# One float32 transformer block on one core: the first MLP product as seven quarter products, on blocks of 768 tokens

## Chip, core and metric

One NeuronCore of a Trainium2 chip runs the whole program. The metric is the device time of one execution in microseconds (us); lower is better. TensorE is called PE below, VectorE DVE, ScalarE ACT, GpSimd POOL; SP (SyncE) only issues transfers.

## What is computed

The reference, cut to its core:

```python
attn = windowed_attention(q, k, v)              # B, H, S, D = 4, 8, 576, 64; window 128, a slope per head
x = attn.transpose(0, 2, 1, 3).reshape(2304, 512)
h = np.maximum(x @ w_in1, 0); x = (h * h) @ w_out1        # w_in 512 x 2048, w_out 2048 x 512
h = x @ w_in2; out = (h * np.cos(h)) @ w_out2
```

All of it is float32. The two MLPs are called layer 1 (relu squared) and layer 2 (h cos h).

## The kernel before

Attention runs first, a pair of heads at a time, 16 pairs, each in a step of a software pipeline. It leaves x transposed on chip: 128 features by 2304 tokens in each of four slabs.

Both MLPs work on blocks of N = 384 tokens, six a layer. Precision is kept by splitting every operand in two fp32r parts: hi (rounded) and lo (the rest). Each product is then three matmuls, hi*hi, hi*lo and lo*hi, summed in PSUM. All of w_in and w_out lies on chip as hi and lo (win_hi, win_lo, wout_hi, wout_lo). The weights of layer 1 are split by POOL during and just after attention, those of layer 2 in place while the last block of layer 1 uses them up (split_weight, L321 to L325: one TENSOR_SCALAR for hi, one TENSOR_TENSOR for lo). Between these two stretches POOL has nothing to do.

A block takes FT = 16 steps f, one for each 128 columns of w_in:

- PE: hidden(t, f), L486 to L499: 4 slabs x 3 = 12 matmuls of 384 columns into one of four PSUM banks. Three steps later second_product (L501 to L533): in layer 1, 12 matmuls of 384 columns; in layer 2, 9 matmuls of 512 columns (tokens are then the output's partitions). They sum over all f in four Y banks.
- Layer 1, relu_step: ACT takes relu of the PSUM tile (L607), DVE multiplies (L780), ACT rounds to g_hi (L602), DVE subtracts to g_lo (L773).
- Layer 2, cos_step: DVE reduces the angle in four instructions (L804, L806, L811, L814; L806 works on what L804 left, L814 on what L811 left), ACT takes Abs and Sin (L624, L626), DVE multiplies by h (L790), ACT rounds (L602), DVE subtracts (L773). L804, L790 and L811 read h from PSUM. The DVE work of two neighbouring f is interleaved in the order written.
- split_x (L591, L764) splits the next block's x; put_y and put_out copy Y to x, whose place SP stores to HBM in layer 2.

Each engine runs its list in the order written; semaphores join them. The order on DVE and ACT was written by hand.

Of the kernel before, what the change touches and what calls it, by code (L numbers as in the profile page):

```python
# [70 lines left out]
ACT_PIECES = [p for p in PIECES if p[0] != 1]  # L71
DVE_PIECES = [p for p in PIECES if p[0] == 1]
# [11 lines left out]
def attention_mlp_kernel(nc, q_t, k_t, v, w_in1, w_out1, w_in2, w_out2, out):  # L84
    with ExitStack() as ctx:
# [21 lines left out]
        wout_raw = place("wout_raw", [P, FT, DM], F32, wout_at)
        wout_end = top[0]

        xs = place("xs", [P, 2, 2, DT, N], F32R)  # L110
        rest_at = [top[0] - 2 * 4 * DT * N]
        rest_end = top[0]
        g_hi = place("g_hi", [P, HID_RING, N], F32R)
        g_lo = place("g_lo", [P, HID_RING, N], F32R)
        work1 = place("work1", [P, 2, N], F32)
        work2 = place("work2", [P, 2, N], F32)
# [5 lines left out]
        probs0 = place("probs0", [P, UNITS, BAND], F32, hi_at)
        pt0 = place("pt0", [P, PT_COLS], F32, hi_at)
        v_raw = place("v_raw", [P, V_RING, 2, 2, 4, D], F32, hi_at)
        v_first = place("v_first", [P, V_RING, D], F32, hi_at)
        slopes = place("slopes", [P, 8], F32, hi_at)
        distance = place("distance", [P, BAND + P], F32, hi_at)
        assert hi_at[0] <= lo_at[0]
        q_raw = place("q_raw", [P, QK_RING, S], F32, lo_at)
        k_raw = place("k_raw", [P, QK_RING, S], F32, lo_at)  # L130
# [17 lines left out]
        H_BANK, Y_BANK = 0, 4  # L148
# [768 lines left out]
```

## Time and profile before

| | us |
|---|---|
| median of three runs | 912.71 (912.64 to 913.2) |
| the profiled execution, its own time | 912.75 |
| its span, first to last instruction | 910.6 |
| PE busy in the span | 894.9 |
| DVE busy | 518.6 |
| ACT busy | 369.2 |
| POOL busy | 193.7 |

Attention fills about the first 110 us, layer 1 goes on to about 510 us, layer 2 to the end. Busy time of an engine says how full it is, not whether anything waits for it; the groups further down are read for that. Durations of single instructions are start to end. Where an engine takes independent instructions one after the other, the next one starts before the record of the last one ends.

### The profile page before, as it was taken

What the parts mean: (1) busy time and instruction counts of PE and PEld (TensorE: products, weight loads), DVE (VectorE), ACT (ScalarE), POOL (GpSimd) and SP (SyncE); (2) the same over time, 40 slices, a digit from 0 to 9 for tenths busy, and PEclk for the clock granted to TensorE, in tenths of its full rate; (3) what the DMA queues carried; (4) which work ended last, traced back from release to release, by engine and by line L of the source; (5) the groups of instructions that cost most, each with busy time, mean ns of one, the idle gap of its engine ahead of it and who ended that gap; (6) DMA issues with size and microseconds to landing.
All of it is one profiled execution on the core that took longest, in us unless ns stands there. A gap on an engine that the chain in (4) does not pass through costs nothing.

```text
span 910.6 us, 17307 instructions
## 1 busy us (share of the span) xinstructions
PE 894.9 (98%) x6128; PEld 840.7 (92%) x6128; DVE 518.6 (57%) x1239; ACT 369.2 (41%) x886; POOL 193.7 (21%) x298
## 2 busy tenths in 40 slices
PE   6999899999999999999999999999999999999998
PEld 4888799999999999999999989999999899999987
DVE  6888553333333332332353878777676776777675
ACT  7888232223232222222232344444444443443433
POOL 9888992000000000000069910000000000000000
PEclk9999999999999999999999999999999999999999
DMA  7776520000000000000134200100100100100101
GB/s 245 251 248 199 165 70 1 1 0 0 0 0 0 0 0 0 0 0 0 46 117 128 80 2 1 35 0 0 35 0 0 35 0 0 35 0 0 35 1 35
DMA packets 22922, 40.15 MB, mean 44 GB/s; under 512 B 3680, under 2 KB 8800, under 8 KB 22880
## 3 DMA queue, kind: packets, MB, share of 16 engines
q1 hardware_dynamic: 22016, 38.77, 13.1%
q10 hardware_dynamic: 864, 0.82, 0.3%
q8 instruction: 26, 0.43, 0.2%
q14 instruction: 16, 0.13, 0.0%
HBM read 34.87 MB, written 4.72 MB: 43 GB/s over the span
## 4 chain that ended last, share of the span: by engine, by line
PE 95%; DVE 2%; POOL 2%; issue 1%; ACT 0%; DVEq 0%; ACTq 0%; POOLq 0%
PE psum L497 43%; PE psum L531 22%; PE psum L516 21%; PE psum L458 4%; PE psum L416 3%; PE psum L370 2%; POOL probs L319 1%; PE psum L379 0%; DVE g_lo L773 0%; DVE work L811 0%; DVE pt L750 0%; POOL win_lo L325 0%; DVE work L804 0%; DVE work L814 0%; POOL bias L309 0%
## 5 line engine op out<-in xcount | busy, mean ns | idle before, releaser
L497 PE MATMUL psum<-xs,win_hi 128*128 (+1 forms) x1536 | 391.6, 335 | 0.0
L497 PEld LDWEIGHTS psum<-xs,win_hi 128*128 128x128 f32 x1536 | 279.4, 188 | 8.4
L497 PE MATMUL psum<-xs,win_lo 128*128 (+1 forms) x768 | 257.8, 336 | 0.0
L602 ACT ACTIVATE g_hi<-work 128x384 fp32r<-128x384 f32 x192 | 101.0, 526 | 218.6 <-DVE work L790 153.9
L773 DVE TENSOR_TENSOR g_lo<-work,g_hi 128x384 fp32r<-128x384 f32 x192 | 119.2, 621 | 57.4 <-ACT g_hi L602 57.4
L780 DVE SCALAR_TENSOR_TENSOR work<-psum,work 128x384 f32<-128x384 f32 x96 | 53.4, 557 | 170.6 <-ACT work L607 170.3
L497 PEld LDWEIGHTS psum<-xs,win_lo 128*128 128x128 f32 x768 | 144.1, 188 | 0.0
L531 PE MATMUL psum<-g_hi,wout_hi 128*128 128x384 f32 x384 | 128.3, 334 | 0.0
L531 PE MATMUL psum<-g_lo,wout_hi 128*128 128x384 f32 x384 | 128.3, 334 | 0.0
L531 PE MATMUL psum<-g_hi,wout_lo 128*128 128x384 f32 x384 | 128.3, 334 | 0.0
L607 ACT ACTIVATE work<-psum 128x384 f32<-128x384 f32 x96 | 47.1, 491 | 193.2 <-PE psum L497 193.2
L516 PE MATMUL psum<-wout_hi,g_lo 128*128 128x512 f32 x288 | 113.9, 396 | 0.0
L516 PE MATMUL psum<-wout_lo,g_hi 128*128 128x512 f32 x288 | 113.7, 395 | 0.0
L516 PE MATMUL psum<-wout_hi,g_hi 128*128 128x512 f32 x288 | 112.0, 389 | 0.3 <-DVE g_lo L773 0.3
L323 POOL TENSOR_SCALAR win_hi<-win_raw 128x512 fp32r<-128x512 f32 x32 | 21.1, 659 | 317.7 <-DMA win_raw<-w_in 317.7
L804 DVE TENSOR_SCALAR work<-psum 128x384 f32<-128x384 f32 x96 | 53.2, 554 | 52.5 <-PE psum L497 52.0
L624 ACT ACTIVATE work<-work 128x384 f32<-128x384 f32 x96 | 50.5, 526 | 57.7 <-DVE work L814 57.7
L531 PEld LDWEIGHTS psum<-g_hi,wout_hi 128*128 128x128 f32 x384 | 72.1, 188 | 0.0
L531 PEld LDWEIGHTS psum<-g_lo,wout_hi 128*128 128x128 f32 x384 | 72.1, 188 | 0.0
L531 PEld LDWEIGHTS psum<-g_hi,wout_lo 128*128 128x128 f32 x384 | 72.1, 188 | 0.0
L579 ACT ACTIVATE probs<-probs,neg_max 128x192 f32<-128x192 f32 (+1 forms) x144 | 61.8, 432 | 12.7 <-DVE neg_max L730 12.7
L516 PEld LDWEIGHTS psum<-wout_hi,g_lo 128*128 128x128 f32 x288 | 54.0, 187 | 11.5
(60 smaller groups left out, 955.5 us busy)
## 6 DMA issues: line engine op xcount, KB each, us to landing
win_raw<-w_in SPq DMA_DIRECT2D x32, 256.0 KB, 3.3
v_raw<-v SPq DMA_DIRECT2D x16, 512.0 KB, 3.2
wout_raw<-w_out SPq DMA_DIRECT2D x32, 256.0 KB, 3.3
q_raw<-q_t SPq DMA_DIRECT2D x15, 288.0 KB, 3.5
k_raw<-k_t SPq DMA_DIRECT2D x15, 288.0 KB, 4.7
out<-x SPq DMA_DIRECT2D x10, 192.0 KB, 1.9
out<-x SPq DMA_DIRECT2D x12, 128.0 KB, 1.7
out<-x SPq DMA_DIRECT2D x10, 64.0 KB, 1.6
```

Source lines behind the costliest of these rows:

```text
L416: return pe.transpose(o[:, at:at + P], of, ident[:])
L458: return pe.matmul(psum[D * h:D * h + D, O_BANK + n % 2, HALF * (n // 2):HALF * (n // 2) + HALF], block, m[block.base_partition():block.ba ...
L497: last = pe.matmul(o, wi[:, f, w], xs[:, bass.ds(par, 1), part, k, :], start=(k == 0 and n == 0), stop=(k == DT - 1 and n == 2))
L516: last = pe.matmul(psum[:, Y_BANK + c, :], g[:, r, tok], w[:, f, :], start=(first and n == 0), stop=(final and n == 2))
L531: last = pe.matmul(psum[:, Y_BANK + d, 0:N], wo[:, f, w], g[:, r, :], start=(first and n == 0), stop=(final and n == 2))
L579: act.activation(m, m, ACT.Exp, bias=neg_max[:, r, u:u + 1], scale=-1.0, accum_out=row_sum[:, r, u:u + 1]).then_inc(exp_ready, 1)
L602: act.activation(g_hi[:, f % HID_RING, :], work2[:, f % 2, :], ACT.Copy).then_inc(g_hi_ready, 1)
L607: act.activation(work1[:, f % 2, :], psum[:, H_BANK + f % HID_RING, 0:N], ACT.Relu)\
L624: act.activation(a, a, ACT.Abs).then_inc(abs_ready, 1)
L773: dve.tensor_tensor(g_lo[:, f % HID_RING, :], work2[:, f % 2, :], g_hi[:, f % HID_RING, :].bitcast(F32), ALU.subtract).then_inc(g_ready, 1)
L780: dve.scalar_tensor_tensor(out=work2[:, f % 2, :], in0=psum[:, H_BANK + f % HID_RING, 0:N], scalar=0.0, in1=work1[:, f % 2, :], op0=ALU.ma ...
L804: dve.tensor_scalar(k, h, 1.0 / (2.0 * math.pi), ROUNDER, ALU.mult, ALU.add).then_inc(angle_steps, 1)
```

## The change

**The product.** x times w_in is now made by Strassen's scheme in Winograd's form. A step n takes a super block of N = 768 tokens (SUPERS = 3 a layer) and two slabs of 128 hidden columns, j and j + 8 (STEPS = 8). w_in's part of the step is cut in quarters A11, A12, A21, A22 (256 input features by 128 hidden columns), x in quarters B11, B12, B21, B22 (256 features by 384 tokens). Seven products (PRODUCTS) of two 128-row slabs each, three matmuls a slab, 384 columns: 42 matmuls of 384 columns a step, 48 steps in all. The four quarter results come from sums of these: some are summed in PSUM, in two banks (H_BANK, i % 2), the rest by five DVE additions of PSUM and an SBUF tile (sum_of) and two ACT copies (copy_part, copy_first_sum). h now lies in SBUF (hidden_sum).

**Operands.** The sums of quarters of x (T1 to T4) are made by DVE (moving_sum, 768 columns each), rounded by ACT (round_moving), their lo parts by DVE (split_moving), once a super block and spread over the steps of the one before. The sums of w_in's quarters (S1 to S4) are made by POOL in each step, rounded by ACT, and their lo parts made by POOL.

**Weights.** Nothing of the weights stays on chip. Each step loads w_in's four quarters (load_raw) and two slabs of w_out (load_wout) again from HBM, and POOL and ACT split them again: for a step POOL has four TENSOR_TENSORs of 256 columns (weight_sums), one of 768 (weights_lo), one of 1024 (sums_lo) and two of 512 (split_wout); ACT has Copies of 768, 1024 and twice 512 columns.

**Order.** PE cuts the second products in pieces (c) and puts them between the seven products by a table (pieces_after). In layer 1 a piece is three matmuls of 512 columns and three of 256, eight a step; in layer 2 it is three of 512, twelve a step. ACT and DVE follow lists of their own (mlp_step). The first MLP step's operands are prepared within attention. At the end three second products (q = 93, 95, 94) are left.

Core of the diff, added lines only (the old functions of these names go):

```diff
+SUPERS = TOKENS // N
+STEPS = FT // 2
+ALL = 2 * SUPERS * STEPS
+W_RING = 4
+FINAL = 2 * ALL - 2
+H_BANK, Y_BANK = 0, 2
+PRODUCTS = ["A11*B11", "S2*T2", "A12*B21", "S3*T3", "S1*T1", "A22*T4", "S4*B22"]
+COMB = ["A22", "A11", "A12", "S1", "S2", "S3", "S4"]
+MOVING = [name.split("*")[1] for name in PRODUCTS]
+MOVING_LO = {"T2": 0, "T3": 1, "T4": 2}
+PLACE = {"B11": (0, 0), "T1": (0, 1), "B12": (0, 1), "B21": (2, 0), "B22": (2, 1)}
+T_STEPS = {"T3": 1, "B11": 2, "T1": 2, "T2": 3, "T4": 4, "B21": 4, "B22": 4}
...
+            def load_raw(n):
+                r, j = n % 2, n % STEPS
+                w_in = w_in2 if second(n) else w_in1
+                if n >= 2:
+                    sp.wait_ge(comb_ready, 2 * (n - 1))
+                sp.dma_start(raw[:, r, 0:2, :], w_in[j + STEPS]).then_inc(raw_landed[r], 16)
+                sp.dma_start(raw[:, r, 2:4, :], w_in[j]).then_inc(raw_landed[r], 16)
+            def load_wout(q):
+                w_out = w_out2 if second(q // 2) else w_out1
+                if q >= W_RING:
+                    sp.wait_ge(second_done, q - W_RING + 1)
+                sp.dma_start(wout_raw[:, q % W_RING, :], w_out[slab(q)]).then_inc(wout_landed[q % W_RING], 16)
...
+            def weight_sums(n):
+                r = n % 2
+                a21, a22, a11, a12 = (raw[:, r, i, :] for i in range(4))
+                pool.wait_ge(raw_landed[r], 32 * (n // 2 + 1))
+                if n > 0:
+                    pool.wait_ge(comb_ready, 2 * n)
+                pool.tensor_tensor(sums[:, 0, :], a21, a22, ALU.add).then_inc(sums_ready, 1)
+                pool.tensor_tensor(sums[:, 2, :], a11, a21, ALU.subtract).then_inc(sums_ready, 1)
+                pool.wait_ge(sums_ready, 4 * n + 1)
+                pool.tensor_tensor(sums[:, 1, :], sums[:, 0, :], a11, ALU.subtract).then_inc(sums_ready, 1)
+                pool.wait_ge(sums_ready, 4 * n + 3)
+                pool.tensor_tensor(sums[:, 3, :], a12, sums[:, 1, :], ALU.subtract).then_inc(sums_ready, 1)
...
+            def weights_lo(n):
+                r = n % 2
+                pool.wait_ge(comb_hi_ready, 2 * n + 1)
+                pool.tensor_tensor(comb_lo[:, r, 0:3, :], raw[:, r, 1:4, :], comb_hi[:, r, 0:3, :].bitcast(F32),
+                                   ALU.subtract).then_inc(comb_ready, 1)
+            def sums_lo(n):
+                r = n % 2
+                pool.wait_ge(comb_hi_ready, 2 * n + 2)
+                pool.tensor_tensor(comb_lo[:, r, 3:7, :], sums[:], comb_hi[:, r, 3:7, :].bitcast(F32),
+                                   ALU.subtract).then_inc(comb_ready, 1)
+            def split_wout(q):
+                r = q % W_RING
+                pool.wait_ge(wout_hi_ready, q + 1)
+                pool.tensor_tensor(wout_lo[:, r, :], wout_raw[:, r, :], wout_hi[:, r, :].bitcast(F32), ALU.subtract)\
+                    .then_inc(wout_ready, 1)
...
+                more = n + 1 < ALL
+                if more:
+                    weight_sums(n + 1)
+                    weights_lo(n + 1)
+                if n > 0:
+                    split_wout(2 * n - 1)
+                if more:
+                    sums_lo(n + 1)
+                split_wout(2 * n)
+            split_wout(2 * ALL - 1)
...
+            def hidden_product(n, i):
+                t, r = n // STEPS, n % 2
+                weight, moving = PRODUCTS[i].split("*")
+                w, m = COMB.index(weight), moving
+                if i < 2:
+                    pe.wait_ge(comb_ready, 2 * n + i + 1)
+                if n % STEPS == 0:
+                    pe.wait_ge(xt_ready, len(MOVING) * t + i + 1)
+                if i == 0 and n > 0:
+                    pe.wait_ge(sum_done, 5 * n)
+                elif i == 2:
+                    pe.wait_ge(part_a_ready, n + 1)
+                elif i == 3:
+                    pe.wait_ge(sum_done, 5 * n + 1)
+                elif i == 4:
+                    pe.wait_ge(first_sum_ready, n + 1)
+                elif i == 5:
+                    pe.wait_ge(sum_done, 5 * n + 2)
+                elif i == 6:
+                    pe.wait_ge(sum_done, 5 * n + 3)
+                first = i in (0, 1, 4)
+                for k in range(2):
+                    cols = slice(k * P, k * P + P)
...
+            def second_product(q):
+                n, r = q // 2, q % W_RING
+                t, start = n // STEPS, q % (2 * STEPS) == 0
+                final = q == FINAL
+                wo, wl = wout_hi[:, r, :], wout_lo[:, r, :]
+                for c in range(6 if second(n) else 4):
+                    if c == 0:
+                        pe.wait_ge(wout_ready, q + 1)
+                        pe.wait_ge(g_ready, 4 * n + (3 if q % 2 else 4))
...
...
+            def pieces_after(n, i):
+                later = second((2 * n - 3) // 2) if i < 4 else second(n - 1)
+                if n % STEPS == 1:
+                    return ((3, 3, 0, 0, 0, 0, 6) if later else (2, 2, 0, 0, 0, 0, 4))[i]
+                return ((2, 1, 2, 1, 2, 2, 2) if later else (1, 1, 1, 1, 1, 1, 2))[i]
+            def mlp_step(n):
+                earlier = second_product(2 * n - 3) if n >= 2 else iter(())
+                later = second_product(2 * n - 2) if n >= 1 else iter(())
+                for i in range(len(PRODUCTS)):
+                    hidden_product(n, i)
+                    for _ in range(pieces_after(n, i)):
+                        next(earlier if i < 4 else later, None)
...
+            def copy_part(n):
+                act.wait_ge(product_done, 7 * n + 1)
+                act.activation(part_a[:], psum[:, H_BANK, 0:NH], ACT.Copy).then_inc(part_a_ready, 1)
+            def copy_first_sum(n):
+                act.wait_ge(product_done, 7 * n + 3)
+                if n > 0:
+                    act.wait_ge(g_done, 4 * (n - 1) + 1)
+                act.activation(hidden_sum[:, 0, :], psum[:, H_BANK, 0:NH], ACT.Copy).then_inc(first_sum_ready, 1)
...
+            def weights_hi(n):
+                r = n % 2
+                act.wait_ge(raw_landed[r], 32 * (n // 2 + 1))
+                if n >= 2:
+                    act.wait_ge(product_done, 7 * (n - 1))
+                act.activation(comb_hi[:, r, 0:3, :], raw[:, r, 1:4, :], ACT.Copy).then_inc(comb_hi_ready, 1)
+            def sums_hi(n):
+                act.wait_ge(sums_ready, 4 * (n + 1))
+                act.activation(comb_hi[:, n % 2, 3:7, :], sums[:], ACT.Copy).then_inc(comb_hi_ready, 1)
...
+            def mlp_step(n):
+                t, j = divmod(n, STEPS)
+                if n > 0:
+                    cosine(n - 1, 3)
+                    if n < ALL:
+                        copy_part(n)
+                    round_g(n - 1, 2)
+                    round_wout(2 * n - 1)
+                if n + 1 < ALL:
+                    weights_hi(n + 1)
+                if n > 0:
+                    round_g(n - 1, 3)
+                if j == 1 and t > 0:
+                    (put_out(t - 1, False) if t > SUPERS else put_y(t - 1))
+                if n == ALL:
+                    return
+                copy_first_sum(n)
+                cosine(n, 0)
+                if n + 1 < ALL:
+                    sums_hi(n + 1)
+                round_g(n, 0)
+                round_wout(2 * n)
+                cosine(n, 1)
+                if t + 1 < 2 * SUPERS:
+                    for name in HI_AT[j]:
+                        round_moving(t + 1, name)
+                round_g(n, 1)
+                cosine(n, 2)
...
+                dve.tensor_tensor(moving_raw(t, name), moving_raw(t, left), moving_raw(t, right), ALU.subtract)\
+                    .then_inc(t_done, 1)
...
+            def sum_of(n, product, bank, left, to):
+                dve.wait_ge(product_done, 7 * n + product + 1)
+                dve.tensor_tensor(to, psum[:, H_BANK + bank, 0:NH], left, ALU.add).then_inc(sum_done, 1)
...
+            def angle(n, i):
+                if not second(n):
+                    return
+                h, k, w = hidden_sum[:, i, :], work1[:, i % 2, :], work2[:, i % 2, :]
+                done = 3 * (4 * (n - ALL // 2) + i)
+                if i == 0:
+                    dve.wait_ge(first_sum_ready, n + 1)
+                else:
+                    dve.wait_ge(sum_done, 5 * n + SUMS_AFTER[i])
+                dve.wait_ge(g_done, 4 * n + i - 1)
                 dve.tensor_scalar(k, h, 1.0 / (2.0 * math.pi), ROUNDER, ALU.mult, ALU.add).then_inc(angle_steps, 1)
+                dve.wait_ge(angle_steps, done + 1)
                 dve.tensor_scalar(k, k, -ROUNDER, None, ALU.add).then_inc(angle_steps, 1)
+                dve.wait_ge(angle_steps, done + 2)
...
+                dve.wait_ge(angle_steps, done + 3)
                 dve.scalar_tensor_tensor(out=k, in0=k, scalar=-TURN_LO, in1=w, op0=ALU.mult, op1=ALU.add)\
                     .then_inc(angle_ready, 1)
...
+            def make_g(n, i):
+                h, w = hidden_sum[:, i, :], work2[:, i % 2, :]
+                if second(n):
+                    dve.wait_ge(cos_ready, 4 * (n - ALL // 2) + i + 1)
+                    dve.tensor_tensor(w, h, work1[:, i % 2, :], ALU.mult).then_inc(g_done, 1)
...
+            def mlp_step(n):
+                t, j = divmod(n, STEPS)
+                if 0 < n < ALL:
+                    part_b_sum(n)
+                if n > 0:
+                    make_g(n - 1, 3)
+                    lo_g(n - 1, 2)
+                if j == 1 and t > 0:
+                    (put_out(t - 1, False) if t > SUPERS else put_y(t - 1))
+                if n < ALL:
+                    angle(n, 0)
+                    part_c_sum(n)
+                if n > 0:
+                    lo_g(n - 1, 3)
+                if n == ALL:
+                    return
+                if t + 1 < 2 * SUPERS:
+                    for name in T_AT[j] if j < len(T_AT) else ():
+                        moving_sum(t + 1, name)
+                    for name in LO_AT[j]:
+                        split_moving(t + 1, name)
+                make_g(n, 0)
+                c22_sum(n)
+                angle(n, 1)
+                lo_g(n, 0)
+                c21_sum(n)
+                make_g(n, 1)
+                angle(n, 2)
+                c12_sum(n)
+                lo_g(n, 1)
+                make_g(n, 2)
+                angle(n, 3)
...
```

## Rows read from the trace of the kernel before

**Rows 1.** The page's first part: busy time of each engine.
```profile
PE 894.9 (98%) x6128; PEld 840.7 (92%) x6128; DVE 518.6 (57%) x1239; ACT 369.2 (41%) x886; POOL 193.7 (21%) x298
```

**Rows 2.** The page's fourth part: the chain that ended last, by engine.
```profile
PE 95%; DVE 2%; POOL 2%; issue 1%; ACT 0%; DVEq 0%; ACTq 0%; POOLq 0%
```

**Rows 3.** Windows (stretch, length, then busy us and count by engine, clock, DMA).
```profile
200.00:300.00 100.00, 100.00 (x579) 100.00 (x578) 31.06 (x56) 27.56 (x56) 0.00 (x0) 1.00 0.00 0
600.00:700.00 100.00, 100.00 (x503) 90.57 (x502) 72.28 (x154) 43.79 (x83) 0.00 (x0) 1.00 0.02 8
```

**Rows 4.** The chain in order of time (start, us, what): runs of matmuls.
```profile
540.47 2.10 PE psum L497 x12
...
898.44 8.22 PE psum L516 x36
```

**Rows 5.** TensorE's timeline in attention, matmuls and their weight loads.
```profile
62.88 0.77 PE L416 MATMUL psum<-ident,probs 128*128 128x128 f32 x5
...
62.87 0.53 PEld L416 LDWEIGHTS psum<-ident,probs 128*128 128x128 f32 x5
```

**Rows 6.** VectorE's timeline (start, us) in layer 2 with POOL idle.
```profile
701.79 0.56 DVE L804 TENSOR_SCALAR work<-psum 128x384 f32<-128x384 f32 x1 [1.25 <-PE psum L497]
702.38 0.36 DVE L806 TENSOR_SCALAR work<-work 128x384 f32<-128x384 f32 x1
702.66 0.55 DVE L790 TENSOR_TENSOR work<-psum,work 128x384 f32<-128x384 f32 x1
703.13 0.54 DVE L811 SCALAR_TENSOR_TENSOR work<-work,psum 128x384 f32<-128x384 f32 x1
703.71 0.56 DVE L814 SCALAR_TENSOR_TENSOR work<-work,work 128x384 f32<-128x384 f32 x1
704.18 0.55 DVE L773 TENSOR_TENSOR g_lo<-work,g_hi 128x384 fp32r<-128x384 f32 x1
```

**Rows 7.** ScalarE's timeline in layer 2: Abs, Sin, and a Copy behind them.
```profile
528.47 0.53 ACT L624 ACTIVATE work<-work 128x384 f32<-128x384 f32 x1 [1.19 <-DVE work L814]
529.03 0.62 ACT L626 ACTIVATE work<-work,half_pi 128x384 f32<-128x384 f32 x1
529.55 0.51 ACT L591 ACTIVATE xs<-x  x1
```

**Rows 8.** Groups by form (count, busy us, mean ns, idle before): ACT copies from PSUM.
```profile
L607 ACT ACTIVATE work<-psum 128x384 f32<-128x384 f32 x96 | 47.1, 491 | 193.2 <-PE psum L497 193.2
...
L588 ACT ACTIVATE pt<-psum 128x512 f32<-128x512 f32 x16 | 9.2, 578 | 9.2 <-PE psum L416 9.2
```

**Rows 9.** VectorE's timeline in layer 2 while POOL splits weights.
```profile
518.09 1.30 DVE L814 SCALAR_TENSOR_TENSOR work<-work,work 128x384 f32<-128x384 f32 x1
519.32 0.96 DVE L773 TENSOR_TENSOR g_lo<-work,g_hi 128x384 fp32r<-128x384 f32 x1
520.20 0.55 DVE L804 TENSOR_SCALAR work<-psum 128x384 f32<-128x384 f32 x1
520.78 0.87 DVE L806 TENSOR_SCALAR work<-work 128x384 f32<-128x384 f32 x1
```

**Rows 10.** POOL's timeline in the same stretch.
```profile
517.69 1.29 POOL L325 TENSOR_TENSOR wout_lo<-wout_raw,wout_hi 128x512 fp32r<-128x512 f32 x1
518.95 0.93 POOL L323 TENSOR_SCALAR wout_hi<-wout_raw 128x512 fp32r<-128x512 f32 x1
519.96 1.48 POOL L325 TENSOR_TENSOR wout_lo<-wout_raw,wout_hi 128x512 fp32r<-128x512 f32 x1
521.40 0.73 POOL L323 TENSOR_SCALAR wout_hi<-wout_raw 128x512 fp32r<-128x512 f32 x1
```

**Rows 11.** Windows: one DVE round of that stretch.
```profile
518.09:522.61 4.52, 4.52 (x25) 4.04 (x24) 4.45 (x6) 1.67 (x4) 4.35 (x5) 1.00 0.00 0
```

**Rows 12.** Windows early in attention (columns as in rows 3).
```profile
16.00:18.00 2.00, 1.19 (x13) 0.94 (x17) 0.68 (x2) 2.00 (x10) 2.00 (x6) 0.84 1.04 391
18.00:20.00 2.00, 2.00 (x34) 1.60 (x28) 0.69 (x5) 1.70 (x7) 1.92 (x5) 0.50 0.42 154
```

More of the change, by code:

```diff
@@ L107, in attention_mlp_kernel @@
[L107 to L116, printed above, removed]
+        x_lo = place("x_lo", [P, DT, TOKENS], F32R, x_at)
+        raw = place("raw", [P, 2, 4, 256], F32)
@@ L122, in attention_mlp_kernel @@
[L122 to L130, printed above, removed]
@@ L484, in values @@
                 last.then_inc(pv_done, 1)
-            def hidden(t, f, second):
-                pe.wait_ge(win_ready, FT * second + f + 1)
-                pe.wait_ge(g_done, step(t, f, 1))
-                o = psum[:, H_BANK + f % HID_RING, 0:N]
-                par = t % 2
-                for k in range(DT):
-                    if f == 0:
-                        pe.wait_ge(xs_ready, t * DT + (k + 1))
-                    w = slice(k * P, k * P + P)
-                    for n, (wi, part) in enumerate(((win_hi, 0), (win_hi, 1), (win_lo, 0))):
-                        last = pe.matmul(o, wi[:, f, w], xs[:, bass.ds(par, 1), part, k, :],
-                                         start=(k == 0 and n == 0), stop=(k == DT - 1 and n == 2))
-                last.then_inc(h_ready, 1)
@@ L640, in put_out @@
+            def put_out(t, final):
+                at = t % SUPERS * N
                 if not final:
-                    act.wait_ge(y_done, step(t, FT - 1, 1 + HID_RING))
-                for c, col, slab, off, w in ACT_PIECES:
+                    act.wait_ge(second_done, 2 * STEPS * (t + 1))
+                for c, col, strip, off, w in ACT_PIECES:
                     if final:
-                        act.wait_ge(last_ready, c + 1)
-                    act.activation(x[:, slab, bass.ds((t - BLOCKS) * N + off, w)], psum[:, Y_BANK + c, col:col + w],
-                                   ACT.Copy).then_inc(out_act, 1)
+                        act.wait_ge(y_done, c + 1)
+                    act.activation(x[:, strip, at + off:at + off + w], psum[:, Y_BANK + c, col:col + w],
+                                   ACT.Copy).then_inc(y_act, 1)
@@ new lines, in part_b_sum, with part_c_sum, c22_sum, c21_sum @@
+            def part_b_sum(n):
+                dve.wait_ge(part_a_ready, n + 1)
+                sum_of(n, 1, 1, part_a[:], part_b[:])
+            def part_c_sum(n):
+                sum_of(n, 3, 1, part_a[:], part_c[:])
+            def c22_sum(n):
+                dve.wait_ge(sum_done, 5 * n + 2)
+                sum_of(n, 4, 0, part_c[:], hidden_sum[:, 1, :])
+            def c21_sum(n):
+                sum_of(n, 5, 1, part_a[:], hidden_sum[:, 2, :])
+            def c12_sum(n):
+                sum_of(n, 6, 0, part_b[:], hidden_sum[:, 3, :])
@@ new lines, in put_out @@
+            def put_out(t, final):
+                at = t % SUPERS * N
+                if not final:
+                    dve.wait_ge(second_done, 2 * STEPS * (t + 1))
+                for c, col, strip, off, w in DVE_PIECES:
+                    if final and c < 5:
+                        dve.wait_ge(y_done, c + 1)
+                    elif final:
+                        dve.wait_ge(second_done, 2 * ALL)
+                    dve.tensor_copy(x[:, strip, at + off:at + off + w], psum[:, Y_BANK + c, col:col + w]).then_inc(y_dve, 1)
```

566 lines of the change are left out of this document (260 added, 306 removed).

## The prediction, made before the changed kernel was run

> **What bounds the kernel now.** First the page's busy shares: PE is busy 98% of the span, DVE 57%, ACT 41%, POOL 21% [rows 1]. Then the chain of waits, which says whether that is a bound: 95% of the chain is PE [rows 2]. Then the windows by stage: in layer 1 and in layer 2 PE is busy 100 of 100 us at full clock, with 579 and 503 matmuls [rows 3]. So a matmul taken off PE is worth its full time, as long as nothing else becomes late. What can become late is read from the same rows: in layer 2 DVE already has 72 of 100 us, and that with POOL doing nothing. 100/579 is 0.173 us for a matmul of 384 columns (12 in 2.10 us on the chain [rows 4]). Layer 2 runs 12 of these and 9 of 512 columns in turn: 21 x 100/503 = 4.17, less 12 x 0.173, leaves 0.233 each; at the end 36 take 8.22, 0.228 each [rows 4]. I take 0.232.
>
> **What goes.** Before, the first products are 192 x 12 = 2304 matmuls of 384 columns, after it 48 x 42 = 2016. 288 x 0.173 = 49.8 us. The second products keep their columns. From the profiled execution's 912.75 us (the median is 912.71) that makes 863 us, if PE never waits.
>
> **256 columns.** In layer 1, 576 matmuls of 512 and 576 of 256 columns replace 1152 of 384. By columns a 256 takes 0.116 and nothing changes. The other end is 0.173, the closest spacing at which fp32r weight loads are seen (578 in 100 us [rows 3]): 576 x 0.057 = 33 us. The five transposes of 128 columns, each with a full weight load, take 0.77 us, their loads 0.53 [rows 5]; less 0.28 and 0.14 for the last one's own length, estimates, that is some 0.12 and 0.10 apart. This row is nearest to a 256, so I take 0 and keep 33.
>
> **A step of PE.** 42 x 0.173 = 7.3, and second products 24 x 0.232 + 24 x 0.116, or 36 x 0.232, = 8.35: 15.6 us in either layer, where the same work took 16.7 before (4 x 4.17). A product is 1.04, a piece 1.04 in layer 1 and 0.70 in layer 2.
>
> **DVE in layer 2, POOL set aside.** Prices from the quiet timeline [rows 6]: an independent instruction of 384 columns starts 0.47 after the one before it (L790 to L811); one that needs the result before it 0.58; SBUF to SBUF with one input (L806) lasts 0.36. So an angle, now all in SBUF and each instruction needing the last, is 0.39 + 0.39 + 0.58 + 0.57 = 1.93. An operation of 768 columns is 0.47 + 0.40 = 0.87; there are 11 in eight steps, 1.2 a step. On ACT, Abs and Sin end 1.2 after the angle and the Copy behind them starts 0.1 before that [rows 7]; Copies are 0.49 for 384 and 0.58 for 512 columns [rows 8], so an estimated 0.8 for 768 and 1.0 for 1024.
> Now the two lists, from the end of angle(n-1, 3) as 0. DVE has nothing until part_b_sum(n), which needs copy_part, which ACT's list puts behind cosine(n-1, 3): it ends at 1.6. part_b_sum, make_g and lo_g run to 3.1. angle(n, 0) needs copy_first_sum, behind round_g, round_wout, weights_hi and round_g on ACT: 4.15. The angle ends at 6.1; part_c_sum, lo_g, moving work, make_g and c22_sum at 9.2; angle 1 at 11.1; lo_g and c21_sum, then make_g(n, 1) waits for the cosine until 12.35; angle 2 ends at 14.75; c12_sum, lo_g; make_g(n, 2) waits until 16.0; angle 3 ends at **18.4**. This chain of DVE and ACT alone is longer than PE's 15.6 and than the 16.7 of before. PE is ahead of it everywhere.
>
> **POOL, which now works all the time.** Rows 9 and 10 show what that does. While POOL's TENSOR_TENSOR runs from 517.69 to 518.98, L814 takes 1.30 instead of 0.56 and ends 0.41 after POOL's; L773 takes 0.96 and ends 0.40 after POOL's next; L806 takes 0.87 instead of 0.36 and ends 0.21 after. POOL in turn takes 0.93 for an instruction that it does in 0.62 to 0.73 otherwise. L804, which reads PSUM, keeps its 0.55 [rows 9, 10]. One round of DVE takes 4.52 there [rows 11], against its own 2.87 (the starts in rows 6 and one more 0.47). So the two take turns, whole instructions at a time, except where DVE reads one operand from PSUM.
> The change takes h out of PSUM: of DVE's 29 instructions of a layer 2 step only the five sums are exempt. POOL has 1.28 for 512 columns, by columns 4 x 0.64 + 1.92 + 2.56 + 2 x 1.28 = 9.6 us a step, behind one another and released by ACT at fixed places. weights_lo starts at 3.3 (after weights_hi) and ends at 5.2; the angle's first instruction (ready at 4.15) ends at 5.45, split_wout (less the 0.13 that it overlaps) at 6.6, the rest of the angle at 8.0: **+1.9**. sums_hi ends at 10.1, sums_lo goes in behind make_g(n, 0) at 10.55 and holds until 13.0; the next angle, ready at 11.1, then alternates with sums_lo, split_wout and two of the next step's weight_sums and ends at 16.4, not at 13.0: **+3.4**. lo_g(n, 0) and c21_sum wait for the last two: **+0.6**, of which 0.4 comes back from the cosine wait. Together 18.4 + 1.9 + 3.4 + 0.6 - 0.4 = **23.9 us a step**. The ends for POOL's share are 0 (18.4) and all of its 9.6 (28.0); I take the walk.
> By the Trainium skill ("SBUF — State Buffer", section on SBUF's two separate sides) VectorE and GpSimd have one pair of ports in common, held for the whole instruction, and the loser is fully blocked; on VectorE's side this counts for two SBUF inputs or a two-port mode. Rows 9 and 10 agree. By that rule the port has a floor of its own: DVE 16 x 0.40 + 8 x 0.21 + 1.1 for the moving work = 9.2, with POOL's 9.6 is 18.8 a step, so under it even the best order is no faster than before.
> PE waits 23.9 - 15.6 = 8.3 in each of 24 steps: **+199**. The last block has no moving work for a next one: 8 x 1.2 = **-10**.
>
> **Layer 1.** DVE's own work is small (5 sums, 8 others of 0.47, 1.2: some 7.4 of 15.6), but PE's slack for each result is 1 to 2.5 us and one POOL instruction holds DVE for up to 2.56. From P0's start as 0: weights_lo holds make_g(n-1, 3) until 5.7, split_wout holds lo_g(n-1, 2) until 7.3, sums_lo (7.7 to 10.2) holds lo_g(n-1, 3) until 10.6. PE wants that at 9.4, for the piece after the fifth product: **+1.2** a step, and 15.6 + 1.2 is no better than 16.7. 22 x 1.2 = **+26** (0 to 60: two such holds). In the second step of each block (pieces 2, 2, 0, 0, 0, 0, 4) five products run with no piece between them, with put_y or put_out, 1.7 to 2.2 us, ahead of the sums that they need: about 2.5 each, five times, **+12** (5 to 25).
>
> **Start and end.** Steps 0 and 1 have no second products to fill in: each of the last products waits for a DVE sum behind moving_sum and a POOL instruction, about 3.5 a step, **+7** (3 to 15). The end loses nothing new: 18 pieces run dense, as 36 matmuls do now. SP streams 1 MB a step, 44 to 67 GB/s, where this trace moved 391 GB/s [rows 12]; its loads are asked for half a step or more ahead of use, so I cost them at nothing. Attention has less POOL work and room on DVE for four instructions: nothing.
>
> **Sum.** 863 + 199 - 10 + 26 + 12 + 7 = **1097 us**.
>
> **Rivals.**
> (a) The turns cost about half, because the lists settle where POOL runs in DVE's waits (1.6 and 1.1 a step) and sums: 21 us a step. 863 + 130 - 10 + 13 + 8 + 6 = 1010. For it: 5 us of a step need no port. Against: POOL starts when ACT releases it, and that is beside an angle.
> (b) No turns at all, DVE and ACT's chain alone: 863 + 24 x 2.8 - 10 + 5 + 5 = 930. Against it: rows 9.
> (c) Faster: PE stays the bound, 863 + 5 + 5 = 873. The place is the wait for copy_part and copy_first_sum; it decides at a DVE round of 15.6. For it: the saved 49.8 us are certain. Against: both waits and the cosine's would have to vanish, and POOL's turns too.
> (d) The clock falls. PE ends its pieces at 15.2 and c12_sum, which frees bank 0, comes at 20.8: 5.6 us of one idle gap a step. In attention PE was busy 1.19 of 2 us, and the granted clock went to 0.84 there and 0.50, 1.2 GHz, in the next stretch [rows 12]. At that level P0, two pieces and P1 take 7 instead of 3.5 us and end 2.2 after DVE wants them: 24 x 2.2 = 53, 1150 us. The Trainium skill ("TensorE: Matmul & The Clock Gate", section on HAM oscillation) says that gaps between bursts do this every round; if it is only a part of the 3.5 us, DVE's slack hides most of it.
> (e) A 256 takes 0.173: PE's layer 1 step is 1.4 longer, which takes some of the waits in. +5 to +33, up to 1130.
>
> **Chances.** The forecast's case (1050 to 1125) 0.48; (a) 980 to 1050, 0.22; (d), or (e) and worse alignment, 1125 to 1200, 0.17; (b) with some waits, 915 to 980, 0.08; (c) 0.04; no change (within 0.2%, what a measurement here can tell) 0.01. Faster 0.04, same 0.01, slower 0.95. For 8 in 10 I give 990 to 1160, which the ends of POOL's share ask for.
>
> **What would show it.** In layer 2: steps of 24 us, DVE busy over 90% with its SBUF instructions at 0.8 to 1.3 us in the mean and sums at 0.55, PE near 65%, its longest wait the first product's for DVE's last sum; DVE's wait for copy_part. In layer 1: steps of 16.5 to 17 and PE waiting for g_lo. PE has 5840 matmuls instead of 6128. Wrong would be: DVE idle while PE is dense, instructions at 0.56 beside POOL's, or 256s spaced 0.17.

## The result

The changed kernel takes 1139.5 us (median of 4 runs, 1138.5 to 1140.3) against 912.7: 1.249 times as long, 95% interval 1.247 to 1.251. Slower was forecast, with 1097 us and a range of 990 to 1160. The time lies in that range, but above the forecast's own case (1050 to 1125).

The page of after, its first part and the head of its fourth (the chain that ended last), to be held against [rows 1] and [rows 2]:

```profile
PE 924.5 (81%) x5840; PEld 812.0 (71%) x5840; DVE 918.4 (81%) x1487; ACT 494.0 (43%) x1055; POOL 602.2 (53%) x563
...
PE 48%; DVE 42%; issue 6%; ACT 3%; POOL 0%; DMA 0%; POOLq 0%; DVEq 0%; ACTq 0%
```

PE has 288 matmuls fewer and is on only 48% of the chain, where it was on 95%; DVE, which was on 2%, is on 42%. POOL and DMA have 0% of it: neither POOL itself nor the loading of the weights is on the chain, so what POOL costs it must cost through another engine. The windows of after, layer 1 and layer 2, answer to [rows 3] (busy us and count of PE, PEld, DVE, ACT, POOL, then clock, DMA share, GB/s):

```profile
300.00:500.00 200.00, 185.97 (x1046) 170.37 (x1045) 159.21 (x169) 74.60 (x131) 125.29 (x95) 0.99 0.20 62
700.00:900.00 200.00, 148.54 (x624) 126.85 (x624) 170.20 (x245) 86.90 (x155) 89.22 (x64) 0.87 0.16 50
```

PE was full in both. Now it is busy 93% in layer 1, 74% in layer 2, and in layer 2 at a clock of 0.87. From one copy_part to the next on ACT's timeline is one step: **17.0 us** in layer 1 in the steps that are no block's first two, **24.9** on average in layer 2 (22.9 to 26.6), against 16.7 before for the same work.

What fills a step of layer 2 is seen on DVE's and POOL's timelines (start, us, engine, line; idle before and what ended it):

```profile
803.65 0.56 DVE L962 SCALAR_TENSOR_TENSOR work<-work,hidden_sum 128x384 f32<-128x384 f32 x1
804.24 0.56 DVE L965 SCALAR_TENSOR_TENSOR work<-work,work 128x384 f32<-128x384 f32 x1
807.60 0.56 DVE L927 TENSOR_TENSOR part_b<-psum,part_a 128x384 f32<-128x384 f32 x1 [2.79 <-PE psum L611]
808.07 0.55 DVE L973 TENSOR_TENSOR work<-hidden_sum,work 128x384 f32<-128x384 f32 x1
808.54 2.21 DVE L986 TENSOR_TENSOR g_lo<-work,g_hi 128x384 fp32r<-128x384 f32 x1
810.66 1.45 DVE L957 TENSOR_SCALAR work<-hidden_sum 128x384 f32<-128x384 f32 x1
812.15 0.36 DVE L959 TENSOR_SCALAR work<-work 128x384 f32<-128x384 f32 x1
...
816.28 2.75 DVE L973 TENSOR_TENSOR work<-hidden_sum,work 128x384 f32<-128x384 f32 x1
```
```profile
808.13 2.20 POOL L407 TENSOR_TENSOR comb_lo<-raw,comb_hi 128x768 fp32r<-128x768 f32 x1 [8.77 <-ACT comb_hi L729]
810.29 1.61 POOL L419 TENSOR_TENSOR wout_lo<-wout_raw,wout_hi 128x512 fp32r<-128x512 f32 x1
815.92 2.70 POOL L413 TENSOR_TENSOR comb_lo<-sums,comb_hi 128x1024 fp32r<-128x1024 f32 x1 [4.03 <-ACT comb_hi L733]
```

lo_g (L986, 0.55 alone) ends at 810.75, 0.42 after weights_lo (L407). The angle's first instruction (L957, 0.36 alone) ends at 812.11, 0.21 after split_wout. make_g (L973, 0.55 alone) ends 0.41 after sums_lo (L413). These are the distances of [rows 9, 10], in other places of the step.

### The profile page after: what moved, and what is told of

It is laid out like the page before. It is cut to its first block, busy times and chain, and to the rows that moved or that the text cites. A ratio compares the mean times of both kernels' runs of the same rounds, so it can differ in the third digit from the quotient of the medians.

```text
span 1137.8 us, 16300 instructions
## 1 busy us (share of the span) xinstructions
PE 924.5 (81%) x5840; PEld 812.0 (71%) x5840; DVE 918.4 (81%) x1487; ACT 494.0 (43%) x1055; POOL 602.2 (53%) x563
## 4 chain that ended last, share of the span: by engine, by line
PE 48%; DVE 42%; issue 6%; ACT 3%; POOL 0%; DMA 0%; POOLq 0%; DVEq 0%; ACTq 0%
PE psum L611 21%; PE psum L638 10%; DVE g_lo L986 9%; DVE work L957 7%; PE psum L633 6%; PE psum L640 5%; DVE work L959 5%; DVE work L962 5%; DVE work L973 4%; DVE work L965 4%; DVE hidden_sum L927 3%; PE psum L557 3%; PE psum L515 2%; PE psum L469 1%; DVE xt_raw L917 1%
## 5 line engine op out<-in xcount | busy, mean ns | idle before, releaser
L611 PE MATMUL psum<-xt_hi,comb_hi 128*128 128x384 f32 x672 | 244.4, 364 | 141.1 <-DVE hidden_sum L927 132.4
L611 PEld LDWEIGHTS psum<-xt_hi,comb_hi 128*128 128x128 f32 x672 | 134.8, 201 | 170.9 <-issue 130.3
L611 PE MATMUL psum<-xt_hi,comb_lo 128*128 128x384 f32 x672 | 237.7, 354 | 0.0
L407 POOL TENSOR_TENSOR comb_lo<-raw,comb_hi 128x768 fp32r<-128x768 f32 x48 | 92.9, 1935 | 257.8 <-ACT comb_hi L729 257.8
L986 DVE TENSOR_TENSOR g_lo<-work,g_hi 128x384 fp32r<-128x384 f32 x192 | 212.9, 1109 | 4.5 <-ACT g_hi L762 0.3
L419 POOL TENSOR_TENSOR wout_lo<-wout_raw,wout_hi 128x512 fp32r<-128x512 f32 x96 | 138.7, 1445 | 111.2 <-ACT wout_hi L740 111.2
L413 POOL TENSOR_TENSOR comb_lo<-sums,comb_hi 128x1024 fp32r<-128x1024 f32 x48 | 117.4, 2446 | 120.8 <-ACT comb_hi L733 120.8
L611 PE MATMUL psum<-x_lo,comb_hi 128*128 128x384 f32 x384 | 139.7, 364 | 0.0
L611 PEld LDWEIGHTS psum<-xt_hi,comb_lo 128*128 128x128 f32 x672 | 135.6, 202 | 0.0
L981 DVE SCALAR_TENSOR_TENSOR work<-hidden_sum 128x384 f32<-128x384 f32 x96 | 114.6, 1194 | 0.0
L611 PE MATMUL psum<-xt_lo,comb_hi 128*128 128x384 f32 x288 | 98.6, 342 | 0.0
L957 DVE TENSOR_SCALAR work<-hidden_sum 128x384 f32<-128x384 f32 x96 | 85.2, 888 | 9.2 <-ACT hidden_sum L722 8.4
L973 DVE TENSOR_TENSOR work<-hidden_sum,work 128x384 f32<-128x384 f32 x96 | 75.5, 786 | 11.6 <-ACT work L754 11.6
```

The costliest lines, as they stand in the source:

```text
L407: pool.tensor_tensor(comb_lo[:, r, 0:3, :], raw[:, r, 1:4, :], comb_hi[:, r, 0:3, :].bitcast(F32), ALU.subtract).then_inc(comb_ready, 1)
L413: pool.tensor_tensor(comb_lo[:, r, 3:7, :], sums[:], comb_hi[:, r, 3:7, :].bitcast(F32), ALU.subtract).then_inc(comb_ready, 1)
L419: pool.tensor_tensor(wout_lo[:, r, :], wout_raw[:, r, :], wout_hi[:, r, :].bitcast(F32), ALU.subtract)\
L611: last = pe.matmul(psum[:, H_BANK + i % 2, 0:NH], wi, mi[:, k, :], start=first, stop=True, skip_group_check=True)
L957: dve.tensor_scalar(k, h, 1.0 / (2.0 * math.pi), ROUNDER, ALU.mult, ALU.add).then_inc(angle_steps, 1)
L973: dve.tensor_tensor(w, h, work1[:, i % 2, :], ALU.mult).then_inc(g_done, 1)
```

## The experiments

Each ran in three rounds beside the kernel before (median 912.0 to 912.5 in these). The step lengths are read as above.

**e1, POOL's work all but taken away**, all else as it is:

```diff
-pool.tensor_tensor(comb_lo[:, r, 0:3, :], raw[:, r, 1:4, :], comb_hi[:, r, 0:3, :].bitcast(F32), ...)
+w = 256 if n < 2 else 8
+pool.tensor_tensor(comb_lo[:, r, 0:3, 0:w], raw[:, r, 1:4, 0:w], comb_hi[:, r, 0:3, 0:w].bitcast(F32), ...)
```
(columns cut in the same way, to 8 or 16, in weight_sums and sums_lo from the third step on, in split_wout from the fifth slab on; wout_raw gets memory of its own; most lo parts of the weights are then stale)

> The changed kernel with POOL's work all but taken away: from the third step on its weight sums and lo parts are made for 8 or 16 columns instead of 256 or 512 (so most of the lo parts are stale, and wout_raw has memory of its own); every wait and order stays. POOL theory (the two engines take turns at whole instructions that touch SBUF twice): layer 2 falls from 24.9 us a step to DVE and ACT's own chain, 18.4 to 18.8, layer 1 from 17.0 to 15.6 to 15.8, 1139 - 24 x 6.3 - 22 x 1.3 = 960 us (935 to 985), and DVE's SBUF instructions are back at 0.36 and 0.56. Rival (DVE is slow for another reason: two SBUF operands as such, or PE's half clock): over 1090, instructions as now.

Measured: 950.7 us, ratio 1.043 (1.041 to 1.045). Steps 15.7 in layer 1, 18.6 on average in layer 2 (18.0 where a step has one moving operation). So POOL's share is 1139.5 - 950.7 = **189 us**; the steps add up to 145 less in layer 2 and 39 less in layer 1. The 189 has in it what the clock cost, for PE's gaps shrink too (mean clock 0.984 against 0.928). DVE's groups by form show it, of after (700 to 900 us) and then of e1 (600 to 900): the instructions on SBUF alone go back to their own lengths, the sum that reads PSUM never left its own.

```profile
L973 DVE TENSOR_TENSOR work<-hidden_sum,work 128x384 f32<-128x384 f32 x32 | 28.5, 891 | 2.4 <-ACT work L754 2.4
L986 DVE TENSOR_TENSOR g_lo<-work,g_hi 128x384 fp32r<-128x384 f32 x32 | 28.4, 888 | 0.0
L957 DVE TENSOR_SCALAR work<-hidden_sum 128x384 f32<-128x384 f32 x32 | 26.4, 824 | 2.6 <-ACT hidden_sum L722 2.4
...
L927 DVE TENSOR_TENSOR part_c<-psum,part_a 128x384 f32<-128x384 f32 x8 | 4.4, 550 | 0.0
```
```profile
L977 DVE TENSOR_TENSOR work<-hidden_sum,work 128x384 f32<-128x384 f32 x65 | 36.3, 558 | 11.2 <-ACT work L758 11.2
...
L990 DVE TENSOR_TENSOR g_lo<-work,g_hi 128x384 fp32r<-128x384 f32 x65 | 36.1, 556 | 0.0
L961 DVE TENSOR_SCALAR work<-hidden_sum 128x384 f32<-128x384 f32 x66 | 23.8, 361 | 15.0 <-ACT hidden_sum L726 14.2
...
L931 DVE TENSOR_TENSOR part_c<-psum,part_a 128x384 f32<-128x384 f32 x16 | 8.8, 551 | 0.0
```

**e2, and no cosine either:** as e1, and angle and cosine return at once, so that make_g takes layer 1's form in both layers.

> As e1, and layer 2's h cos h is replaced by layer 1's relu squared, so that DVE and ACT have little to do. If the seven products are worth what was predicted and 256 column matmuls cost nothing extra, PE is the bound in both layers at 15.6 us a step: 863 + 5 to 20 for start and block ends = 875 (865 to 890), 38 us under the kernel before. Rival (the seven products bring less, by waits between their two banks or by weight loads): 16 or more a step, over 895.

Measured: 884.4 us, ratio 0.970 (0.968 to 0.971). The windows of e2, a stretch of each layer:

```profile
150.00:480.00 330.00, 328.66 (x1886) 306.05 (x1885) 165.05 (x308) 136.93 (x236) 37.73 (x168) 1.00 0.21 67
500.00:860.00 360.00, 358.69 (x1784) 321.03 (x1783) 171.11 (x326) 142.31 (x251) 39.89 (x173) 1.00 0.23 73
```

PE is full and the steps are 15.7 us (a block's second step 16.0 to 16.9). So the seven products do give what they promise; the cosine's chain on DVE and ACT takes 950.7 - 884.4 = **66 us**. e2 lies 21 us over the 863 of a PE that never waits, 9 over what was expected. About 12 of the 21 lie in the first two steps and the end, the rest in steps of 15.65 and in the blocks' second steps.

**e3, useless matmuls in PE's gap:**

```diff
+if n > ALL // 2:
+    ...                                  # the waits of the first product
+    pe.wait_ge(sum_done, 5 * n - 1)      # c21_sum: bank 1 is free
+    for _ in range(20):
+        pe.matmul(psum[:, H_BANK + 1, 0:NH], comb_hi[:, n % 2, 0, 0:P], moving_hi(n // STEPS, "B11")[:, 0, :], ...)
```

> The changed kernel with 20 useless matmuls of 384 columns a step in layer 2, in PE's gap while it waits for c12_sum, into the bank that is free. Clock theory (the gap drops the granted clock, and P0, the pieces and P1 after it run at half speed while DVE waits for them): the clock is 1.0 throughout layer 2 and DVE's wait for part_b_sum falls by 1.2 us a step, 1139 - 29 = 1110 (1095 to 1125). Rival (DVE is the bound and PE's speed is hidden): within 5 of 1139.

Measured: 1128.9 us, 10.6 under after and short of the 29 expected; the mean clock of the run rises from 0.928 to 0.964. In layer 2 (700 to 900 us) it is 0.95 and not the 1.0 expected: PE still waits 1.7 us on average for c21_sum ahead of the useless matmuls. The gap is there in after, on PE's timeline. The first product waits 5.07 us for c12_sum and then starts its matmuls 0.32 apart (802.22 to 802.54), 384 columns at 1.2 GHz, until the second product, where they are 0.17 apart again:

```profile
801.77 0.66 PE L611 MATMUL psum<-xt_hi,comb_hi 128*128 128x384 f32 x1 [5.07 <-DVE hidden_sum L927]
802.22 0.52 PE L611 MATMUL psum<-x_lo,comb_hi 128*128 128x384 f32 x1
802.54 0.52 PE L611 MATMUL psum<-xt_hi,comb_lo 128*128 128x384 f32 x1
...
806.27 0.35 PE L611 MATMUL psum<-xt_hi,comb_hi 128*128 128x384 f32 x1
806.46 0.34 PE L611 MATMUL psum<-xt_lo,comb_hi 128*128 128x384 f32 x1
```

In e3 DVE's wait before part_b is still 2.47 us in some steps, where the dummies stand before the product, and in 14 of 23 steps it is the one that the prediction named, for part_a:

```profile
798.56 0.56 DVE L935 TENSOR_TENSOR part_b<-psum,part_a 128x384 f32<-128x384 f32 x1 [2.47 <-PE psum L611]
...
823.54 0.56 DVE L935 TENSOR_TENSOR part_b<-psum,part_a 128x384 f32<-128x384 f32 x1 [1.62 <-ACT part_a L723]
```

How much of the 29 the dummies themselves took was not measured; the clock is worth at least 10.6 us.

**e4, the kernel before with POOL made busy** in 72 of layer 2's 96 rounds:

```diff
+pool.wait_ge(y_done, HID_RING + step(t, f, 1))
+for _ in range(4):
+    ...                                  # each waits for the one before it
+    pool.tensor_tensor(scratch[:], wout_hi[:, 0, 0:256].bitcast(F32), wout_hi[:, 1, 0:256].bitcast(F32), ALU.subtract)...
```

> The kernel BEFORE, with POOL made busy in 72 of layer 2's 96 rounds: four TENSOR_TENSORs of 256 columns a round on a scratch tile, 2.56 us per 4.18, the same share as the change asks for. Theory (only instructions with no PSUM operand take turns with POOL): three of DVE's six are blocked, the round grows from 2.87 by some 1.3 to about 4.2, so PE's 4.18 still bounds: 912 to 928 us. Rival (POOL slows all of DVE): 5.4 a round, 912 + 72 x 1.2 = 1000.

Measured: 912.0 us, ratio 1.000 (0.999 to 1.001). DVE's groups of e4 between 600 and 800 us: L786, L827 and L819 have no PSUM operand, L824 has one.

```profile
L786 DVE TENSOR_TENSOR g_lo<-work,g_hi 128x384 fp32r<-128x384 f32 x48 | 44.3, 923 | 0.0
L827 DVE SCALAR_TENSOR_TENSOR work<-work,work 128x384 f32<-128x384 f32 x48 | 41.7, 870 | 1.6
...
L824 DVE SCALAR_TENSOR_TENSOR work<-work,psum 128x384 f32<-128x384 f32 x48 | 26.0, 542 | 0.0
...
L819 DVE TENSOR_SCALAR work<-work 128x384 f32<-128x384 f32 x47 | 25.6, 545 | 1.6
```

POOL was busy 75% of these 200 us and DVE 92%, and PE waited for nobody. POOL work at the rate that the change asks for (2.56 us in PE's 4.18), in three quarters of the rounds, costs the old kernel nothing, if by little: DVE's round has 8% left. The changed kernel loses 145 us in layer 2 by its POOL work.

**e9 and e10, where h lies.** In the kernel before, the three DVE instructions that read h from PSUM read a fixed SBUF tile; e10 is that with e4's POOL work.

```diff
-h = psum[:, H_BANK + f % HID_RING, 0:N]
+h = win_hi[:, 0, 0:N].bitcast(F32)          # and the same in cos_g; DVE first waits for that tile's split
```

> The kernel BEFORE; in layer 2 DVE's three instructions that read h from PSUM (L804, L811, L790) read a fixed SBUF tile instead (so its output is not h cos h), nothing else. POOL is idle there. Own lengths stay 0.36 to 0.56, DVE's round stays near 2.7, PE's 4.18 bounds: 912 (910 to 914) under every theory; it is the control for e10.

> e9 with e4's POOL work (four TENSOR_TENSORs of 256 columns a round, 72 rounds). e4 cost nothing because three of DVE's six instructions read PSUM. If the SBUF operand in their place is what costs, all six take turns with POOL: 2.7 + 2.56 less the 0.13 overlap of each = 4.8 a round against PE's 4.18, 72 x 0.6 = +40, 955 (930 to 985). Rival (where h lies does not matter; the change's longer lists and waits did it): 912 as e4.

Measured: e9 918.1 us, ratio 1.006 (1.005 to 1.008); e10 967.0, ratio 1.061 (1.059 to 1.063). The control came out 4 us over its range, and for the same cause: its PE waits 4.7 us for g_lo in all, where layer 2 starts with POOL still splitting weights and DVE busy 9.9 of each 10 us (510 to 530). With h in SBUF POOL's work costs 967.0 - 918.1 = 49 us, with h in PSUM nothing (e4). The windows of e10 show PE with 13% idle, at full clock:

```profile
600.00:700.00 100.00, 87.23 (x425) 75.86 (x424) 93.18 (x129) 37.10 (x71) 72.55 (x83) 1.00 0.02 8
```

**e11, POOL writes but reads nothing:** e4 with eight memsets of 256 columns a round for the four TENSOR_TENSORs.

> e4 with POOL's work exchanged for eight memsets of 256 columns a round, which read nothing. The time is 912 either way; the question is DVE's lengths. If only POOL instructions that read SBUF block DVE's two-operand ones, L814 and L773 stay at 0.56 beside them; if any POOL instruction does, they grow as in e4 (0.87 and 0.92).

Measured: 912.4 us. POOL is busy 2.9 us of each 4.19, and DVE's instructions beside it keep their lengths, L826 0.56 and L785 0.55 (0.87 and 0.92 in e4). POOL's timeline and DVE's in e11 (its first line is an L818 of an earlier round, with memsets beside it from 648.08 on):

```profile
702.50 2.90 POOL L372 MEMSET scratch<- 128x256 f32 x8 [1.29 <-PE psum L528]
```
```profile
648.38 0.60 DVE L818 TENSOR_SCALAR work<-work 128x384 f32<-128x384 f32 x1
...
702.88 0.55 DVE L785 TENSOR_TENSOR g_lo<-work,g_hi 128x384 fp32r<-128x384 f32 x1
704.67 0.56 DVE L816 TENSOR_SCALAR work<-psum 128x384 f32<-128x384 f32 x1 [1.24 <-PE psum L509]
705.26 0.36 DVE L818 TENSOR_SCALAR work<-work 128x384 f32<-128x384 f32 x1
```

**e5 to e8, the order of the lists.** e5 puts copy_part(n) ahead of cosine(n-1, 3) on ACT; e6 is e5 with e3's matmuls; e7 puts weights_hi(n+1) and round_wout(2n-1) at the head of ACT's step; e8 has all of them and pieces (1, 1, 1, 1, 0, 2, 2) in layer 1.

```diff
 # e7, on ACT's list (conditions left out)
+weights_hi(n + 1)
+round_wout(2 * n - 1)
 cosine(n - 1, 3)
 copy_part(n)
 round_g(n - 1, 2)
-round_wout(2 * n - 1)
-weights_hi(n + 1)
```

> The changed kernel, one exchange on ACT's list: copy_part(n) ahead of cosine(n-1, 3). The prediction held DVE's wait for part_b_sum to be one for copy_part (1.6 us). The trace of after names PE instead: the second product, at half clock, comes 1.2 us after part_a is there. If that is right the exchange is worth nothing: 1134 to 1140. If copy_part is what DVE waits for: 24 x 1.6 less, 1100.

> e3 (clock kept up by useless matmuls) and e5 together. With the clock up DVE's wait is in most steps one for part_a, so now the exchange should bring what it does not bring alone: 1 to 1.2 us a step against e3's 1129, 1103 (1095 to 1115). If DVE is held by POOL alone: 1129 as e3.

> The changed kernel, ACT's weights_hi(n+1) and round_wout(2n-1) moved to the head of its step, ahead of cosine(n-1, 3), so that POOL does weights_lo and the first split_wout (3.2 us) while DVE waits for PE anyway. The work of every engine is the same. Alignment theory (what counts is where POOL's instructions fall): lo_g's 2.2 us and the angle's first 1.45 us go back to 0.55 and 0.36, 2.5 a step in layer 2, 1139 - 60 = 1080 (1060 to 1100), and in layer 1 some of PE's 1.3 a step may go too. Rival (POOL's microseconds cost the same wherever they fall): within 10 of 1139.

> e3, e5, e7 and, in layer 1, the piece after the fifth product put one product later (pieces 1, 1, 1, 1, 0, 2, 2), which takes PE's 1.1 us wait for g_lo away: 22 x 1.1 = 24 less by itself. If all four add up: 1139 - 10 - 25 - 60 - 24 = 1020 (1000 to 1045). If the port is a floor that order can't pass, layer 2 stays over 22 us a step and the whole over 1070. The kernel before is not reached in either case.

Measured: e5 1134.7, e6 1124.9, e7 1110.9, e8 1079.9 us (ratios 1.245, 1.234, 1.218, 1.187). e5 came out as the trace said: with the clock low, part_a is not what DVE waits for. e6 missed: 4 us under e3, not 26. e7 missed too: 29 under after, half of what was expected, and most of it in the other layer (the steps of layer 1 fall to 16.2 and 16.7 and add up to 17 less, those of layer 2 to 10 less). DVE's timeline and POOL's in e7 show why: weights_lo and split_wout no longer hold lo_g and the next angle's start, they hold the last angle instead.

```profile
805.13 0.35 DVE L959 TENSOR_SCALAR work<-hidden_sum 128x384 f32<-128x384 f32 x1
805.52 1.96 DVE L961 TENSOR_SCALAR work<-work 128x384 f32<-128x384 f32 x1
807.51 1.52 DVE L964 SCALAR_TENSOR_TENSOR work<-work,hidden_sum 128x384 f32<-128x384 f32 x1
```
```profile
805.43 1.83 POOL L407 TENSOR_TENSOR comb_lo<-raw,comb_hi 128x768 fp32r<-128x768 f32 x1 [3.81 <-ACT comb_hi L729]
807.22 1.39 POOL L419 TENSOR_TENSOR wout_lo<-wout_raw,wout_hi 128x512 fp32r<-128x512 f32 x1
```

e8 missed its 1020 (1000 to 1045) and came out as its other case had it: layer 2 over 22 us a step, the whole over 1070. Layer 1's steps outside a block's first two are 15.7 in e8, PE's own, with all of POOL's work there, so what layer 1 lost in these was a matter of order alone (a block's second step is still 18.9, against 16.8 in e1). Layer 2's stay at 23.6 on average. Nothing tried on the order, with or without useless matmuls, took more than 1.3 us off them, and e1, the work gone, took 6.3. That the two engines' turns are a floor under layer 2 which no order passes is not shown; only these orders were tried. No version that computes the cosine reaches the kernel before: e1's 18.6 a step, with POOL out of the way, is already over its 16.7.

## Why the prediction held, step by step

The mechanism held: POOL's work turns DVE's lists into the bound of layer 2. The time came out 42 us over the 1097, in the stretch (1125 to 1200) that the prediction kept, with a chance of 0.17, for a lower clock (d), or (e) and worse alignment; the lower clock was there. Where the 42 lie is said term by term.

- **The bound and the 49.8 us.** Held: e2 runs both layers at PE's 15.7 a step (15.6 predicted).
- **256 columns at 0.116.** Held: a matmul of 256 is followed by the next after 0.11 to 0.12 us on PE's timeline of after (362.98 to 363.09), weight loads and all, and layer 1's step without POOL is 15.65 (e1, e2), where (e) would have made it 17. The same lines show the wait of layer 1, 1.09 us for g_lo behind the fifth product, predicted as 1.2 in that place; under them stand DVE's instruction that ends it, and sums_lo, which holds that one as the prediction said (it ends 0.41 after):

```profile
361.25 0.33 PE L611 MATMUL psum<-xt_hi,comb_lo 128*128 128x384 f32 x1
362.67 0.47 PE L638 MATMUL psum<-g_hi,wout_hi 128*128 128x512 f32 x1 [1.09 <-DVE g_lo L986]
362.98 0.28 PE L640 MATMUL psum<-g_hi,wout_hi 128*128 128x256 f32 x1
363.09 0.39 PE L638 MATMUL psum<-g_lo,wout_hi 128*128 128x512 f32 x1
```
```profile
360.01 2.51 DVE L986 TENSOR_TENSOR g_lo<-work,g_hi 128x384 fp32r<-128x384 f32 x1
```
```profile
359.72 2.39 POOL L413 TENSOR_TENSOR comb_lo<-sums,comb_hi 128x1024 fp32r<-128x1024 f32 x1 [0.80 <-ACT comb_hi L733]
```

- **DVE and ACT's chain, 18.4 a step.** Held: e1 has 18.6 on average, and DVE waits there where the prediction had it, 1.6 us for part_a and 1.0 for copy_first_sum in most steps. The prediction spread the moving work evenly (1.2 a step); it falls into the first half of a block, where e1's steps are 19 to 21. The last block, which has none, takes 17.8 a step against 19.0 in the two before it: 9 us less, for 10 predicted. These averages contain the blocks' second steps, for which 7.5 of the +12 were meant. So 24 x 18.6 = 446 stand against 24 x 18.4 - 10 + 7.5 = 439: **7 us** short.
- **POOL's turns, +5.5 net.** The mechanism is shown three ways: taken from the changed kernel (e1), given to the old one (e4), and given to the old one with h in SBUF (e10). Its size is 24.9 - 18.6 = 6.3 a step, 0.8 more than the prediction gave: **19 us** short. Its second hold is there in size, and in some steps in place, as here: the second angle takes 5.5 us, from 842.72 to 848.19, instead of 1.9 (+3.4 was said).

```profile
842.72 2.08 DVE L957 TENSOR_SCALAR work<-hidden_sum 128x384 f32<-128x384 f32 x1
844.84 1.33 DVE L959 TENSOR_SCALAR work<-work 128x384 f32<-128x384 f32 x1
```

  In others sums_lo falls on make_g (2.75 at 816.28) and less on the angle. The first hold (+1.9 on the angle's start) falls on make_g and lo_g too, since DVE comes later than predicted: at 807.60 and again at 834.24 it has waited 2.8 and 3.3 us for the second product. So the sum is better than its places, and in that there is some luck. Part of the 19 is most likely rival (d), which the sum left out: the clock falls in PE's gap, as it said, and costs at least 10.6 us (e3). Its worst case, 53, had the second product at half speed as well; the trace has only the first product and its pieces there. What the clock costs in full is open.
- **Where DVE waits.** Wrong in after: it waits 2.8 us for the second product (PE), not 1.6 for copy_part. The 1.6 appears where the clock is kept up (e3) and in e1. Two of the signs are off too: PE is busy 74% of layer 2 and not near 65, DVE 85% and not over 90. Matmuls at half clock and DVE's longer wait for them fit both.
- **Layer 1.** 17.0 instead of 16.8 a step, 4 us; with the blocks' second steps (19.4 and 20.9) **5 us** short.
- **Start and end.** The remaining **11 us** or so. Steps 0 and 1 had 3.5 each for waiting. The mechanism is the one named, a DVE sum behind moving_sum and a POOL instruction, but the last product of step 0 waits 5.1 us for c22_sum, held up behind these two instructions of DVE, and then the granted clock is 0.50 (120 to 128 us):

```profile
116.06 2.46 DVE L917 TENSOR_TENSOR x<-x 128x768 f32<-128x768 f32 x1
118.44 2.69 DVE L981 SCALAR_TENSOR_TENSOR work<-hidden_sum 128x384 f32<-128x384 f32 x1
```
```profile
121.74 0.66 PE L611 MATMUL psum<-xt_hi,comb_hi 128*128 128x384 f32 x1 [5.12 <-DVE hidden_sum L927]
```

- **Rival (a)**, that the lists settle where POOL's work falls in DVE's waits, is what e7 tried to bring about, and it did not in layer 2. **(b)** is e1: 930 said, 951 measured. **(c)** fell with [rows 9] already. **(e)** fell by e1 and e2.

Put together: products -28 net of start and block ends (912.7 to 884.4), cosine's chain +66, POOL +189 with the clock's share in it.

## What to carry over

Before work is taken off the full engine, add up the next one's list at its own start to start distances, with what each instruction waits for; here DVE and ACT needed 18.4 us where PE needed 15.6. Ask of every operand that moves from PSUM to SBUF who else uses that way: three of DVE's six instructions were safe from POOL only because they read PSUM. An engine that was idle (POOL, between the weight splits) is not free to use when it shares a path with the one that becomes the bound, and where two engines take turns and one of them is the bound, another order mostly moves the collision (layer 2 of e7); where it is not the bound, order can hide it (layer 1 of e8).

## What the chip showed that was not expected

- A POOL instruction that only writes (memset) does not hold up DVE's two-operand instructions: 0.55 to 0.56 beside POOL busy 2.9 us of 4.19 (e11), against 0.87 to 0.92 beside instructions that read SBUF (e4). The Trainium skill ("SBUF — State Buffer", on the two separate sides) makes this exception, and e11 agrees. Its one-operand instruction is another case. L818's mean is 0.375 there, but most of its runs meet no memset or only the last 0.14 us of one. Of the six that lay wholly beside memsets one took 0.36 and five 0.44 to 0.60, so a memset can hold it up.
- In the step shown the clock is back 4.5 us after PE's restart at 801.77: from 806.27 on the matmuls are 0.17 apart. Useless matmuls in the gap more than paid for themselves (e3, 10.6 us), though DVE's lists were the bound.
